# The first batch of an attention stage changes to the form of the later batches: folded scores, paired products with the values, rounding moved between engines

## What is computed

```
B, H, S, D = 4, 8, 576, 64
scores = q @ k.T / sqrt(D) - slope[head] * |i - j|     # where 0 <= i - j < 128, else -1e9
attn   = softmax(scores);   out = attn @ v
```

## Time and profile before

| | |
|---|---|
| median of 3 runs | 2034.33 us (2033.43 to 2035.38) |
| the profiled execution | 2034.47 us, span from first to last instruction 2032.7 us |
| PE busy | 2021.0 us (99%) |
| DVE busy | 1289.6 us (63%) |
| ACT busy | 791.7 us (39%) |
| POOL busy | 1305.8 us (64%) |
| the chain that ended last, by engine | PE 95%, DVE 2%, ACT 1%, POOL 1% |
| first scores to first product of the network | 4.30 to 49.31 us |

### The profile page before, as it was taken

The page is one execution under the profiler, slowest core; times in us unless marked ns, Lnnn a source line. Parts: engine busy times, 40 slices in busy tenths (PEclk is TensorE's granted clock), DMA queues, the critical chain, the costliest instruction groups (busy, mean ns, idle before and its releaser), DMA issues.

```text
span 2032.7 us, 35864 instructions
## 1 busy us (share of the span) xinstructions
PE 2021.0 (99%) x11800; PEld 1856.8 (91%) x11800; DVE 1289.6 (63%) x2700; ACT 791.7 (39%) x1571; POOL 1305.8 (64%) x1883
## 2 busy tenths in 40 slices
PE   9999999999999999999999999999999999999999
PEld 6999999999989999999998999999999989999998
DVE  8877868755585655565566556555666565565555
ACT  7665656544324333332343233233333332332331
POOL 5445455564576666667776666766867766667663
PEclk9999999999999999999999999999999999999999
DMA  5544445322122222222222222222223222222221
GB/s 152 128 114 119 123 103 128 78 75 81 54 63 73 62 72 62 72 71 63 74 94 73 62 72 65 69 64 70 72 63 104 62 73 62 72 67 67 67 67 62
DMA packets 178081, 161.45 MB, mean 79 GB/s; under 512 B 28992, under 2 KB 127808, under 8 KB 177984
## 3 DMA queue, kind: packets, MB, share of 16 engines
q1 hardware_dynamic: 177696, 159.93, 28.2%
q10 hardware_dynamic: 288, 0.30, 0.0%
HBM read 155.47 MB, written 4.72 MB: 79 GB/s over the span
## 4 chain that ended last, share of the span: by engine, by line
PE 95%; DVE 2%; ACT 1%; POOL 1%; issue 0%; DMA 0%; ACTq 0%; DVEq 0%; SPq 0%
PE bank L936 38%; PE bank L882 34%; PE bank L815 9%; PE bank L822 9%; PE bank L806 1%; PE bank L768 1%; PE bank L780 1%; PE bank L764 1%; POOL xw L630 1%; PE bank L738 0%; POOL wl L607 0%; PE bank L788 0%; DVE xl L1299 0%; DVE prob L1278 0%; ACT prob L1017 0%
## 5 line engine op out<-in xcount | busy, mean ns | idle before, releaser
L692 POOL TENSOR_TENSOR el<-ew,eh 128x256 fp32r<-128x256 f32 x672 | 472.4, 739 | 294.4 <-ACT eh L1001 294.4
L1451 DVE SCALAR_TENSOR_TENSOR z_sb<-bank,gate,z_sb 128x512 f32<-128x512 f32 x540 | 404.0, 749 | 251.9 <-PE bank L936 251.9
L882 PE MATMUL bank<-xh,eh 128*128 128x384 f32 x1344 | 450.4, 335 | 0.0
L882 PE MATMUL bank<-xh,el 128*128 128x384 f32 x1344 | 450.2, 335 | 0.0
L936 PE MATMUL bank<-fh,gl 128*128 128x512 f32 x1152 | 450.1, 391 | 0.0
L936 PE MATMUL bank<-fl,gh 128*128 128x512 f32 x1152 | 450.0, 391 | 0.0
L882 PE MATMUL bank<-xl,eh 128*128 128x384 f32 x1344 | 449.6, 335 | 0.0
L936 PE MATMUL bank<-fh,gh 128*128 128x512 f32 x1152 | 449.1, 390 | 0.4 <-DVE z_sb L1442 0.4
L702 POOL TENSOR_TENSOR fl<-fw,fh 128x256 fp32r<-128x256 f32 x384 | 276.9, 752 | 137.2 <-ACT fh L1001 136.7
L1001 ACT ACTIVATE p<-bank 128x384 f32<-128x384 f32 x96 | 47.2, 492 | 669.0 <-PE bank L882 669.0
L607 POOL TENSOR_TENSOR wl<-stage,wh 128x256 fp32r<-128x256 f32 x256 | 199.6, 801 | 140.2 <-ACT wh L1001 139.0
(11 more groups left out here) (126 smaller groups left out, 2929.9 us busy)
## 6 DMA issues: line engine op xcount, KB each, us to landing
fw<-in_moe_w_dram SPq DMA_DIRECT2D x96, 512.0 KB, 3.7
ew<-in_moe_w_dram SPq DMA_DIRECT2D x96, 256.0 KB, 2.8
stage<-in_moe_w_in_dram SPq DMA_DIRECT2D x64, 256.0 KB, 2.9
stage<-in_moe_w_out_dram SPq DMA_DIRECT2D x64, 256.0 KB, 2.7
a<-in_moe_w_dram SPq DMA_DIRECT2D x96, 128.0 KB, 2.6
ew<-in_moe_w_dram SPq DMA_DIRECT2D x96, 128.0 KB, 2.9
acc<-in_k_dram SPq DMA_DIRECT2D x24, 288.0 KB, 4.5
acc<-in_q_dram SPq DMA_DIRECT2D x24, 288.0 KB, 4.6
```

What stands on the lines that cost most here:

```text
L692: last = pool.tensor_tensor(el[r][:, a, :, :], ew[r][:, a, :, :], f(eh[r][:, a, :, :]), ALU.subtract)
L882: done = pe.matmul(ps, w[r][:, a, kc, :], x[:, b, kc, :], start=(first and kc == 0 and w is eh and x is xh), stop=(kc == 1 and w is el), s ...
L1451: dve.scalar_tensor_tensor(out=z, in0=ps, scalar=weight, in1=z, op0=ALU.mult, op1=ALU.add).then_inc(z_free, 1)
```

## The change

The first batch takes the folded form. `fold` makes a predicated copy for each of the two heads' banks (128 columns each) in blocks with two key tiles; bias, exponentials, scaling and transposes become 128 columns wide (two transposes a block instead of four); `part_tiles` on POOL parts the triangles. The first batch's order of PE in a slot becomes that of the later ones, `attend` ahead of `transpose_p`, and `attend` is done for two blocks at a time (`group(0)` = 2), in the even slots; ACT and DVE read out both blocks with one copy and one difference in the slot after, ahead of `p_copy` on ACT. One `rouse` product a slot instead of two from slot 3 on. The rounding of the eight weight pieces moves from POOL to ACT, and the pieces come after slots 8, 9, 11, 13, 14, 16, 18 and 19. The biases of heads 2 to 7 are made by ACT in slots 1 to 3 (a scaled copy of the distances). The tile `ring` goes: the distances' first half is overwritten with the maximum of both halves, ahead of the first bias.

Not shown below: the removed tile and semaphores, the removed function `columns`, the wait of the second `l1` on `pT_copied` instead of `pT_out`, and waits that have no longer a purpose. Lines without a mark say in which function a part stands.

```diff
+        def group(b):
+            return GROUP if b else GROUP // 2
         def attended(b, j):
...
-            n = j - OUT_LAG
-            if b == 0:
-                return [n] if 0 <= n < STEPS else []
-            return list(range(n - GROUP + 1, n + 1)) if n >= 0 and (n + 1) % GROUP == 0 else []
+            n, size = j - OUT_LAG, group(b)
+            return list(range(n - size + 1, n + 1)) if n >= 0 and (n + 1) % size == 0 else []
...
         def read_out(b, j):
...
-            blocks = attended(b, j if b == 0 or j == SLOTS - 1 else j - 1)
+            blocks = attended(b, j if j == SLOTS - 1 else j - 1)
...
         def o_part(blocks, nq):
...
+        PIECE_SLOTS = (8, 9, 11, 13, 14, 16, 18, 19)
         def alone_events():
...
-                if j % 2 and j // 2 < PIECES:
-                    ev.append(("w", j // 2))
+                if 0 <= j - PE_LAG < STEPS:
+                    ev.append(("part", 0, j - PE_LAG))
+                if j in PIECE_SLOTS:
+                    ev.append(("w", PIECE_SLOTS.index(j)))
...
-            pool.wait_ge(dist_ready, 1)
-            pool.wait_ge(bias_ready, 2)
-            for h in range(2, H):
-                pool.tensor_scalar(bias[:, h, :], dist[:, :], float(2.0 ** (-8.0 * (h + 1) / H)) / SCALE, MASKED / SCALE,
-                                   ALU.mult, ALU.max).then_inc(bias_ready, 1)
...
             def piece_lo(n, s, i):
...
-                difference(s, i)
-            def piece_both(i, s, uses, seen):
-                wait_alone(pool, w_in[i % 2], uses)
-                pool.tensor_copy(wh[s][:, i, :], stage[:, i % 2, :]).then_inc(w_hi2, 1)
-                pool.wait_ge(w_hi2, seen + (i + 1))
...
             def mixture(p, i, t):
...
             def stretch(events, n0, u0):
...
-                    if what == "w" and u0 == 0:
-                        piece_both(a[0], 0, (a[0] // 2 + 1) * 16, 0)
-                    elif what == "w":
+                    if what == "w":
...
             def transpose_p(b, j, n):
-                nq, k0 = span(j % QT)
-                if b:
-                    if b > 1 or j:
-                        pe.wait_ge(pT_copied, (b - 1) * STEPS + j)
-                    wait_alone(pe, norm_done, b * STEPS + (j + 1))
-                    ps = pT_ps[0][:, 0:2 * P].rearrange("p (h n) -> p h n", h=2)
-                    for h in range(2):
-                        last = pe.transpose(ps[:, h, :], prob_of(b, j)[:, h, 0:P], ident[:, :])
-                    last.then_inc(pT_done, 1)
-                    return
-                bank_wait(pT_out, b, j, n)
+                if b or j >= n:
+                    pe.wait_ge(pT_copied, b * STEPS + (j - n + 1))
...
-                ps = pT_ps[(j + 1) % n][:, :].rearrange("p (k h n) -> p k h n", h=2, k=2)
-                for kt in range(k0 // P, 2):
-                    for h in range(2):
-                        last = pe.transpose(ps[:, kt, h, 0:nq], prob_of(b, j)[0:nq, h, kt * P:(kt + 1) * P],
-                                            ident[0:nq, 0:nq])
+                ps = pT_ps[(j + 1) % n][:, 0:2 * P].rearrange("p (h n) -> p h n", h=2)
+                for h in range(2):
+                    last = pe.transpose(ps[:, h, :], prob_of(b, j)[:, h, 0:P], ident[:, :])
...
             def attend(b, j):
...
-                if b == 0:
-                    bank_wait(x_lo, b, j, 1)
-                elif j % GROUP == 0:
+                if j % group(b) == 0 and b + j:
...
-                            rouse((0, 2, 4)[j] if j < 3 else 2)
-                        if ba == 0 and 0 <= j - PE_LAG < STEPS:
-                            transpose_p(ba, j - PE_LAG, n)
+                            rouse((0, 2, 4)[j] if j < 3 else 1)
...
-                        if ba and 0 <= j - PE_LAG < STEPS:
+                        if 0 <= j - PE_LAG < STEPS:
...
-                    p = prob_of(b, j)[0:nq, h, columns(b, j)]
+                    p = prob_of(b, j)[0:nq, h, 0:P]
...
             def p_copy(b, j, n):
-                ks, nq = slice(0 if j % QT else 1, 2), span(j % QT)[0]
+                nq, _ = span(j % QT)
...
-                if b:
-                    ps = pT_ps[0][:, 0:2 * P].rearrange("p (h n) -> p h n", h=2)
-                    copy(pT[:, j % GROUP, 1, :, 0:nq], ps[:, :, 0:nq]).then_inc(pT_copied, 1)
-                    return
-                ps = pT_ps[(j + 1) % n][:, :].rearrange("p (k h n) -> p k h n", h=2, k=2)
-                copy(pT[:, j % GROUP, ks, :, 0:nq], ps[:, ks, :, 0:nq]).then_inc(pT_out, 1)
+                ps = pT_ps[(j + 1) % n][:, 0:2 * P].rearrange("p (h n) -> p h n", h=2)
+                copy(pT[:, j % GROUP, 1, :, 0:nq], ps[:, :, 0:nq]).then_inc(pT_copied, 1)
...
             def o_hi(b, blocks, written):
...
+            def steep_bias(first):
+                act.wait_ge(ring_ready, 1)
+                for h in (first, first + 1):
+                    copy(bias[:, h, :], dist[:, :], float(2.0 ** (-8.0 * (h + 1) / H)) / SCALE).then_inc(bias_later, 1)
...
             def stretch(events, n16, u0, w=None):
...
-                        if b == 0 and 0 <= j - PE_LAG < STEPS:
-                            p_copy(b, j - PE_LAG, bufs(b))
+                        if b == 0 and j in (1, 2, 3):
+                            steep_bias(2 * j)
...
-                        if b and 0 <= j - PE_LAG < STEPS:
+                        if 0 <= j - PE_LAG < STEPS:
...
-                    if what == "w" and w is not None:
+                    if what == "w":
...
+            dve.tensor_tensor(dist[:, 0:P], dist[:, 0:P], dist[:, P:], ALU.max).then_inc(ring_ready, 1)
+            dve.wait_ge(ring_ready, 1)
...
-            dve.tensor_tensor(ring[:, :], dist[:, 0:P], dist[:, P:], ALU.max).then_inc(ring_ready, 1)
...
             def split_lo(b, c, r):
...
-            def fold(b, j):
+            def fold(b, j, n):
...
-                if not k0:
+                if k0:
+                    return
+                folds[0] += 1
+                if folds[0] == 1:
+                    dve.wait_ge(older_ready, 1)
+                if b == 0:
+                    for bank_of_head in (s_ps, s_odd):
+                        one = bank_of_head[j % n][0:nq, 0:2 * P]
+                        last = dve.copy_predicated(one[:, P:], older[0:nq, 0, :].bitcast(mybir.dt.uint32), one[:, 0:P])
+                else:
...
-                    folds[0] += 1
-                    dve.copy_predicated(both[:, :, 1, :], older[0:nq, :, :].bitcast(mybir.dt.uint32),
-                                        both[:, :, 0, :]).then_inc(folded, 1)
+                    last = dve.copy_predicated(both[:, :, 1, :], older[0:nq, :, :].bitcast(mybir.dt.uint32),
+                                               both[:, :, 0, :])
+                last.then_inc(folded, 1)
...
             def biased(b, j, n, h):
...
-                if b:
-                    if h == 0 and not k0:
-                        dve.wait_ge(folded, folds[0])
-                    last = dve.tensor_tensor_reduce(
-                        out=prob_of(b, j)[0:nq, h, 0:P], in0=s_ps[0][0:nq, (2 * h + 1) * P:(2 * h + 2) * P],
-                        in1=dist[0:nq, P:2 * P] if k0 else ring[0:nq, :], scale=-1.0 / steepness(head), scalar=3.0e38,
-                        op0=ALU.add, op1=ALU.min, accum_out=negmax[0:nq, j % 2, h:h + 1])
-                    if h:
-                        last.then_inc(neg_done, 1)
-                    return
-                if h == 0:
-                    wait_alone(dve, s_done, b * STEPS + (j + 1))
-                if plain(b) and h == 0 and j % QT == 0:
-                    dve.wait_ge(bias_ready, 2 * (j // QT) + 2)
-                scored = (s_ps, s_odd)[h][j % n][0:nq, k0:2 * P]
+                if h == 0 and not k0:
+                    dve.wait_ge(folded, folds[0])
+                if b == 0 and h == 0 and k0:
+                    if j:
+                        dve.wait_ge(bias_later, head)
+                    else:
+                        dve.wait_ge(bias_ready, 2)
+                if b == 0:
+                    scored, distances, scale = (s_ps, s_odd)[h][j % n][0:nq, P:2 * P], bias[0:nq, head, :], -SCALE
+                else:
+                    scored, distances = s_ps[0][0:nq, (2 * h + 1) * P:(2 * h + 2) * P], dist[0:nq, :]
+                    scale = -1.0 / steepness(head)
...
-                    out=prob_of(b, j)[0:nq, h, k0:], in0=scored,
-                    in1=bias[0:nq, head, k0:], scale=-SCALE, scalar=3.0e38,
-                    op0=ALU.add, op1=ALU.min, accum_out=negmax[0:nq, j % 2, h:h + 1])
+                    out=prob_of(b, j)[0:nq, h, 0:P], in0=scored, in1=distances[:, P:] if k0 else distances[:, 0:P],
+                    scale=scale, scalar=3.0e38, op0=ALU.add, op1=ALU.min, accum_out=negmax[0:nq, j % 2, h:h + 1])
...
-                if mine and b:
-                    fold(b, j)
-                if mine and not b:
-                    biased(b, j, n, 0)
+                if mine:
```

(21 more changed lines are left out.)

## The result

The changed kernel took 2044.16 us (median of 6 runs, 2042.67 to 2045.22) against 2034.18 (6 runs): ratio 1.0048, interval 1.0035 to 1.0061. It is 10 us slower. The forecast was 2040.4 within 2033 to 2045. The profiled execution took 2045.22, its span is 2043.5 us (before 2034.47 and 2032.7).

What follows compares the result with a forecast made beforehand. The pace passes from PE to a circle through all engines: 3.5 us for a later `l1` and longer slot 22, with 2.5 of POOL's 6.0, on the profiled 2034.47: 2040.4 us, range 2033 to 2045.

Steps and rivals of the forecast that it cites:

- The circle: First batch: waits from DVE's read-out through PE, ACT and DVE pace two slots at 4.42 us, before 4.2; chance 0.55.
- The start and the end: Transposes of slot 4 start at about 13.4 us; `l1` follows 2.7 us after the transposes of slot 20.
- The even pieces: Weight rounding on ACT after slots 8, 14, 16 and 18 delays the exponentials: 4 x 0.52 = 2.1 us.
- POOL beside DVE: POOL's selects and differences lengthen DVE's sums and scalings: 2.0 us with even pieces, 0.5 in the other four circles.
- the row of 0.60: DVE scaling beside a POOL select takes 0.60 against 0.48, so a select met costs 0.12, not its whole 0.41.
- The clock: PE's granted clock: a fall was priced only as an alternative, up to 13 us in the stage, outside the forecast sum.
- Rival 4: PE idles more and its clock falls: 2053 over the stage, 2043 if only after the last wait; chance 0.10.
- Rival 3: PE's own order paces the first batch at 1.8 us a slot, total 2030.5 or 2028; chance 0.13.

Runs made afterwards that it cites:

- experiment 1: Changed kernel plus six rouse products ahead of the attends of each even slot from 4 on, ten more before `l1`: 2039.80 us.
- Experiment 3: Changed kernel with the first batch's transposes issued ahead of the attends again: 2033.17 us.
- experiment 2: Changed kernel with two rouse products a slot from slot 3 on instead of one: 2040.56 us.
- experiment 4: Changed kernel with the eight weight pieces after odd slots 5 to 19 only: 2040.04 us.
- experiment 6: Changed kernel with rouse products added in PE's waits and weight pieces after odd slots only: 2037.53 us.
- experiment 9: Changed kernel with rouse products added in PE's waits and half of POOL's differences left out for the first eight pieces: 2038.46 us.
- experiment 7: Changed kernel with transposes ahead of attends, two rouse products a slot and six more in each of slots 20 and 21: 2033.58 us.
- experiment 8: Changed kernel with transposes first, two rouse products a slot, six more in slots 20 and 21, pieces after odd slots 5 to 19: 2033.12 us.
- experiment 5: Kernel before the change with only the first batch's transposes moved behind the attend: 2043.68 us.

## Why the prediction was right, and where it was off

The side, the range and the cause were right; the size was short by 3.8 us of 10.

- **The circle.** Its pieces stand in the trace of after as worked out: 0.14, two attends, transposes, copy, exponentials, sums, biases, scalings, read-out. With the clock held (experiment 1) eight circles take 38.0 us, predicted 38.7 with POOL's part. `o_lo` of two blocks was taken at 0.42 and is 0.41; the two folds at 0.51 and are 0.47 to 0.49. Experiment 3 takes one link out of the circle and the whole loss goes, most of the clock's share with it, since PE's waits are shorter: that shows the cause.
- **The start and the end.** Transposes of slot 4 were predicted at 13.4 and start at 13.38. In that there is luck: the two profiled executions get to full speed at about 11 us both; in experiments 1, 2 and 4, where it comes at about 4.4 us, the same work is there at 12.53. (The kernel before starts it at 13.02, not at the 12.9 of the prediction.) From the transposes of slot 20 to `l1` 2.7 were predicted, and 2.67 passed (54.59 to 57.26).
- **The even pieces.** 2.1 predicted; 2.0 in the circles and 2.3 in the total between experiments 1 and 6. Right.
- **POOL beside DVE.** 2.5 predicted, 2.0 of it in the circles of even pieces. The sum without POOL is 36.2, and experiment 1 took 38.0; with the odd pieces it is 34.1, and experiment 6 took 36.0. So some 1.9 are there, near the 2.5, but they don't go away when no piece is even. The largest part is in the circle from slot 10 to slot 12, 4.8 instead of 4.2, where two scalings take 1.13 beside POOL's selects and difference against 0.48 without POOL. The second scaling's piece of the chain in experiment 1, first without, then with POOL's difference:

```profile
15.46 0.27 DVE prob L1258
...
28.91 0.81 DVE prob L1258
```

  With half of the differences left out (experiment 9) this pair still takes 1.12, so the 0.4 of that experiment isn't the price of POOL. The prediction read the row of 0.60 as speaking against a wait for POOL's whole instruction; in experiment 9 this pair ends 0.08 after POOL's difference, so that isn't settled. In the circle from slot 4 to slot 6, 4.8 instead of 4.4, DVE stands for 0.41 for which the profile names no cause.
- **The clock.** This is the term that was mis-sized. Rival 4 was priced as an alternative to the forecast, with 0.10, and the forecast itself put the clock at nothing; it came on top, with about 4 us between after and experiment 1. In the profiles the eight circles take 3.2 more, and the first products of `l1` 1.4 more. The prediction saw the two places (less busy PE, the wait before `l1`) and judged by a mean of 80% busy. The falls came in or just behind waits of 1.2 to 1.9 us, but waits as long passed without one, and what decides isn't shown. The Trainium skill ("TensorE: Matmul & The Clock Gate", section "Part 1: The HAM clock gate (the "warmup" mystery)") says that the half clock is the default and that activity releases it. Experiment 1 agrees (1.000 in all its runs, with more activity), and experiment 2 adds that one dummy product more in each slot makes falls rarer (0.997 to 1.000 instead of 0.994 to 0.996) without ending them.
- **Rival 3** (PE's order paces, 2030.5) decides under 3.6 us for two slots. Even with the circle open they take 4.1, so it didn't come.
- **Where the gain of the narrower tiles went.** PE's transposes and rouse products are fewer, ACT's instructions shorter. None of it set the pace: experiments 3, 7 and 8 keep the narrow tiles, without the circle and (7, 8, in their profiles) without clock falls, and end where the kernel before is. DVE gained narrower biases and scalings and paid with the folds, and with scalings that POOL's selects and differences lengthen. No version tried beats the kernel before clearly.

## What to carry to other kernels

When a change moves an instruction past another in one engine's queue, follow the new wait through all engines until it comes back; a circle of short links sets the pace even where no engine is busy for its whole length. Price the clock as a part of such a forecast, not as its rival: where a circle makes PE wait for over 1 us at a time, the clock can fall though PE is busy for most of the stage. And check which engine is second before cutting work on the first: here DVE stood at 91% behind PE's 95%.

## What the runs showed of the hardware

- The granted clock fell to 0.50 in or just behind waits of PE of 1.2 to 1.9 us (after and experiments 2 to 5), in stages in which PE was busy for some 70 to 90% on average, with one or two extra products a slot, and also in the kernel before with only its transposes moved (experiment 5). Once, in the changed kernel, it fell some 1.6 us behind the end of a wait. Waits of 1.6 us in the changed kernel and of 2.2 in experiment 2 were followed by none.
- Six dummy products (some 0.8 us) put ahead of each pair of attends, where waits had been up to 1.9 us long, and ten ahead of `l1`, kept it at 1.000 in all six runs and made the kernel about 4 us faster than without them.
- When PE gets to full speed at the start differs between executions of nearly the same queue: at 4.4 us in one, after 14 us in another, worth 2.7 us at slot 4, with the granted clock reading 1.00 throughout. It may be a large part of the scatter of 3 us between runs; two profiles don't show how large.
